# A fused attention and two-FFN kernel: the order of the loads and of the work in its first two tiles

## What is computed

```python
def _attn_ref(q, k, v, n_global, n_local):        # q, k, v: (2, 8, 768, 64)
    scores = matmul(q, k.T) / sqrt(64)
    keep = (pos_k < n_global) | ((rel >= 0) & (rel < n_local))      # 8 and 96
    scores = scores - slope[h] * dist ; scores = where(keep, scores, -1e9)
    return matmul(softmax(scores), v)             # softmax with + 1e-9 in the sum

def _moe_ref(x, w_in, w_out, g_ln):               # 512 -> 1024 -> 512
    h = x @ w_in
    solu = h * softmax(h)
    ln = (solu - mean) / sqrt(var + 1e-6) * g_ln
    return ln @ w_out

def _moe2_ref(x, w_gate, w_val, w_out, rms_g):    # 512 -> 1536 -> 512
    xn = x / rms(x) * rms_g
    return (silu(xn @ w_gate) * (xn @ w_val)) @ w_out
```

## Time and profile before

| what | value |
|---|---|
| time, median of 3 runs | 598.04 us (596.92 to 598.3) |
| span of the profiled execution, first to last instruction | 596.7 us |
| PE busy | 566.4 us, 95% of the span |
| DVE, ACT, POOL busy | 305.0, 258.1, 74.6 us |
| DMA | 46.95 MB, mean 79 GB/s |

### The profile page before, as it was taken

How to read it: one execution, slowest core, us unless ns; L and a number is a source line. 1 busy time by engine, 2 the same in 40 slices (tenths; PEclk the granted TensorE clock), 3 DMA queues, 4 the chain that set the end, 5 groups by cost and what they waited for, 6 DMA issues and landing times.

```text
span 596.7 us, 10660 instructions
## 1 busy us (share of the span) xinstructions
PE 566.4 (95%) x3696; PEld 511.4 (86%) x3696; DVE 305.0 (51%) x786; ACT 258.1 (43%) x597; POOL 74.6 (13%) x215
## 2 busy tenths in 40 slices
PE   2488999999999999999999999999999999999997
PEld 1477888888888888878899999999999999999996
DVE  5478788777877898868455223222222222231211
ACT  2566756655665677646454212221222222222112
POOL 1240220222112205213010010001001000100000
PEclk9998799999999999999999999999999999999999
DMA  7676464433443343232532100010020000000000
GB/s 171 185 192 163 132 182 125 121 101 101 124 113 103 105 126 96 83 135 82 176 109 93 49 23 2 1 70 1 1 70 0 0 0 35 0 0 36 2 1 36
DMA packets 22965, 46.95 MB, mean 79 GB/s; under 512 B 4128, under 2 KB 4128, under 8 KB 22928
## 3 DMA queue, kind: packets, MB, share of 16 engines
q1 hardware_dynamic: 22928, 46.48, 26.8%
HBM read 40.18 MB, written 6.29 MB: 78 GB/s over the span
## 4 chain that ended last, share of the span: by engine, by line
PE 78%; DVE 9%; DMA 3%; issue 3%; POOL 3%; ACT 2%; SPq 1%; ACTq 0%; DVEq 0%
PE hidden L396 9%; PE hidden L397 8%; PE hidden L398 8%; PE mixed L1211 5%; PE mixed L396 3%; PE mixed L397 3%; PE scores_b L396 3%; PE scores_b L397 3%; PE scores_b L398 3%; PE mixed L398 3%; PE turned L396 3%; PE turned L397 3%; PE scores_a L397 3%; PE turned L398 3%; PE scores_a L396 3%
## 5 line engine op out<-in xcount | busy, mean ns | idle before, releaser
L708 ACT ACTIVATE act_hi<-act_sb 128x256 fp32r<-128x256 f32 x72 | 30.1, 418 | 108.7 <-DVE act_sb L1070 108.7
L1211 PEld LDWEIGHTS mixed<-v_in,probs_t 116*128 116x128 f32 x384 | 55.3, 210 | 14.5 <-ACT probs_t L659 10.8
L1211 PE MATMUL mixed<-v_in,probs_t 116*128 116x64 f32 x384 | 54.2, 289 | 9.8 <-ACT probs_t L659 9.8
L1070 DVE TENSOR_TENSOR act_sb<-mixed,silu 128x256 f32<-128x256 f32 x36 | 15.3, 425 | 93.7 <-PE mixed L398 93.1
L1070 DVE TENSOR_TENSOR act_sb<-turned,silu 128x256 f32<-128x256 f32 x36 | 15.3, 424 | 89.0 <-PE turned L398 86.5
L396 PE MATMUL hidden<-down_hi,act_hi 128*128 128x512 f32 x144 | 57.0, 396 | 0.1
L397 PE MATMUL hidden<-down_lo,act_hi 128*128 128x512 f32 x144 | 56.9, 395 | 0.0
L398 PE MATMUL hidden<-down_hi,act_lo 128*128 128x512 f32 x144 | 56.7, 394 | 0.0
L659 ACT ACTIVATE probs_t<-turned 116x512 f32<-116x512 f32 x48 | 28.7, 597 | 60.7 <-PE turned L1196 60.7
L1075 DVE TENSOR_TENSOR act_lo<-act_sb,act_hi 128x256 fp32r<-128x256 f32 x72 | 30.6, 425 | 34.9 <-ACT act_hi L708 34.9
L649 ACT ACTIVATE probs<-logits,neg_max 128x232 f32<-128x232 f32 x96 | 45.7, 482 | 5.8 <-DVE neg_max L961 5.8
(11 more groups left out here) (140 smaller groups left out, 1537.2 us busy)
## 6 DMA issues: line engine op xcount, KB each, us to landing
qk_raw<-qk_pairs SPq DMA_DIRECT2D x96, 180.0 KB, 3.5
v_in<-v_windows SPq DMA_DIRECT2D x12, 464.0 KB
staging<-w_gate SPq DMA_DIRECT2D x3, 1024.0 KB, 6.5
staging<-w_val SPq DMA_DIRECT2D x3, 1024.0 KB, 5.5
y_spill<-y_out SPq DMA_DIRECT2D x12, 256.0 KB, 8.4
staging<-w_down SPq DMA_DIRECT2D x3, 1024.0 KB, 5.5
y_in<-y_spill SPq DMA_DIRECT2D x6, 512.0 KB, 3.7
out<-o_sb SPq DMA_DIRECT2D x12, 256.0 KB, 2.1
```

The costliest lines, as they stand in the source:

```text
L708: nc.scalar.activation(act_hi[:, slot], act_sb[:, slot], ACT.Copy).then_inc(act_rounded, 1)
L1070: nc.vector.tensor_tensor(act_sb[:, slot], val_ps[slot][:, 0:WIDE], silu[:, slot], ALU.mult).then_inc(act_ready, 1)
L1211: ins = pe.matmul(mixed[:, head * d:(head + 1) * d], probs_t[:, p % 2, h, half], v_in[:, even, half, head * d:(head + 1) * d], start=(half ...
```

## The change

The changed kernel computes the same with the same instructions, but for three things. The scales are loaded as rows (12 rows of 128 floats), PE transposes them once and ACT copies them to columns (`gain_cols`). The values come in two DMAs for each tile, of 112 and 4 partitions. And the lists are in another order at the beginning:

- SP loads all four pairs of tile 0 first, then the values, block 0, two pairs of tile 1, block 1. The bounds and the scales are issued by ACT, on its own queue, ahead of ACT's first instruction.
- Blocks 0 and 1 of `w_in` are no longer rounded and split one half after each pair of tile -1. Block 0 is done whole after its last pair, block 1 whole after the first pair of tile 0, and block 2's halves one pair later than before.
- PE no longer makes the scores of n = 4 inside tile -1. At the head of tile 0 it now transposes `x`, makes the scores of n = 4, and then all 12 products of `ffn_in(0, ..., 0, ...)`, before the pairs of tile 1 go on. ACT and DVE have the matching steps there. Products for n = 1 stay at pair 2 of tile 0.

```diff
-        round_1 = {(-1, 0): [(0, 0)], (-1, 1): [(0, 1)], (-1, 2): [(1, 0)], (-1, 3): [(1, 1)],
-                   (0, 0): [(2, 0)], (0, 1): [(2, 1)], (1, 0): [(3, 0)], (1, 1): [(3, 1)],
+        round_1 = {(-1, 3): [(0, 0), (0, 1)], (0, 0): [(1, 0), (1, 1)],
+                   (0, 1): [(2, 0)], (0, 2): [(2, 1)], (1, 0): [(3, 0)], (1, 1): [(3, 1)],
...
+        split_1[-1, 3] = split_1.pop((0, 0))
...
-                sp.dma_start(v_in[:, even], v_windows[a].rearrange("p (a n) -> p a n", a=2)
-                             ).then_inc(v_loaded[even], 16)
+                window = v_windows[a].rearrange("p (a n) -> p a n", a=2)
+                for rows in (slice(0, V_ROWS), slice(V_ROWS, HALF)):
+                    sp.dma_start(v_in[rows, even], window[rows]).then_inc(v_loaded[even], 16)
...
-            for i, n in enumerate((n_global, n_local)):
-                sp.dma_start(bounds_i[:, i, :], n.bitcast(I32).partition_broadcast(P)).then_inc(bounds_in, 16)
-            load_qk(0, 0)
-            load_qk(0, 1)
+            for p in range(pairs):
+                load_qk(0, p)
             load_v(0, 0)
             load_block(sp, 0)
-            load_qk(0, 2)
-            load_qk(0, 3)
+            load_qk(1, 0)
+            load_qk(1, 1)
             load_block(sp, 1)
-            with nc.allow_non_contiguous_dma(reason="the gains as columns"):
-                sp.dma_start(gln_col[:], g_ln.rearrange("(k p) -> p k", p=P)).then_inc(cols_loaded, 16)
-                sp.dma_start(rms_col[:], rms_g.rearrange("(k p) -> p k", p=P)).then_inc(cols_loaded, 16)
...
+            for i, n in enumerate((n_global, n_local)):
+                act.dma_start(bounds_i[:, i, :], n.bitcast(I32).partition_broadcast(P)).then_inc(bounds_in, 16)
+            act.dma_start(gain_rows[0:K1], g_ln.rearrange("(k p) -> k p", p=P)).then_inc(gains_loaded, 16)
+            act.dma_start(gain_rows[K1:], rms_g.rearrange("(k p) -> k p", p=P)).then_inc(gains_loaded, 16)
             round_qk(0, 0)
             round_qk(1, 1)
+            act.wait_ge(gains_turned, 1)
+            nc.scalar.activation(gain_cols[:], turned_x[:, 0:K1 + KM], ACT.Copy).then_inc(cols_ready, 1)
             exp_pair(0, 0, 0)
...
+                    if known(t) and t == 0 and p == 0:
+                        turn_x(t)
+                        score_pair(n, p)
+                        ffn_in(t, even, 0, range(0, KM))
                     score_pair(n + 1, (p + 1) % pairs)
...
             pe.wait_ge(ident_done, 1)
+            pe.wait_ge(gains_loaded, 32)
+            pe.transpose(turned_x[:, 0:K1 + KM], gain_rows[:], ident[0:K1 + KM, 0:K1 + KM]).then_inc(gains_turned, 1)
             score_pair(0, 0)
```

More of the change, by code:

```diff
@@ L33 @@
 HALF = WIN // 2
+V_ROWS = 112
 MASKED = 1e30
@@ L358, in round_block @@
                 return
-            act.wait_ge(cols_loaded, 32)
             for k in ks:
@@ L498, in one_tile @@
                 for p in range(pairs):
-                    if is_tile(a + 1):
+                    first = known(t) and t == 0
+                    if first and p == 0:
+                        finish_x(t, general)
+                    if is_tile(a + 1) and not (known(t) and t < 0 and p < 2):
                         load_qk(a + 1, p)
-                    if p == 1 and is_tile(t):
+                    if p == 1 and is_tile(t) and not first:
                         finish_x(t, general)
@@ L732, in one_tile @@
                     n = pairs * a + p
+                    if known(t) and t == 0 and p == 0:
+                        round_x(t, even)
+                        round_qk(n, p)
+                        round_qk(n + 1, p + 1)
+                        exp_pair(n, 1 - even, p)
                     if p == 2 and is_tile(t - 1):
                         round_ln(t - 1, 0)
-                    round_qk(n + 2, (p + 2) % pairs)
+                    if not (known(t) and t < 0 and p >= 2):
+                        round_qk(n + 2, (p + 2) % pairs)
                     if known(t) and t == tiles - 1 and p == 3:
@@ L740, in one_tile @@
                     copy_turned(n, p)
-                    if p == 0 and is_tile(t):
+                    if p == 0 and is_tile(t) and not (known(t) and t == 0):
                         round_x(t, even)
@@ L746, in one_tile @@
                         copy_y(t - DRAIN, even)
-                    exp_pair(n + 1, 1 - even if p < pairs - 1 else even, (p + 1) % pairs)
+                    if not (known(t) and t < 0 and p == 3):
+                        exp_pair(n + 1, 1 - even if p < pairs - 1 else even, (p + 1) % pairs)
                     for c, half in round_1.get((t, p), ()) if known(t) else ():
@@ L1083, in one_tile @@
                         normalise_x(t, even)
+                    if known(t) and t == 0 and p == 0:
+                        split_x(t, even)
+                        split_qk(n, p)
+                        split_qk(n + 1, p + 1)
+                        take_logits(n, 1 - even, p)
                     if p == 3 and is_tile(t):
                         max_hidden(t, 1)
-                    take_logits(n + 1, 1 - even if p < pairs - 1 else even, (p + 1) % pairs)
+                    if not (known(t) and t < 0 and p == 3):
+                        take_logits(n + 1, 1 - even if p < pairs - 1 else even, (p + 1) % pairs)
                     if p == 0 and is_tile(t - 1):
@@ L1094, in one_tile @@
                         max_hidden(t, 0)
-                    split_qk(n + 2, (p + 2) % pairs)
-                    if p == 0 and is_tile(t):
+                    if not (known(t) and t < 0 and p >= 2):
+                        split_qk(n + 2, (p + 2) % pairs)
+                    if p == 0 and is_tile(t) and not (known(t) and t == 0):
                         split_x(t, even)
@@ L1204, in mix_pair @@
                 if p == 0:
-                    pe.wait_ge(v_loaded[even], 16 * (a // 2 + 1))
+                    pe.wait_ge(v_loaded[even], 32 * (a // 2 + 1))
                 if p == 0 and (not known(a) or a >= 1):
@@ L1320, in one_tile @@
                         turn_pair(n, p)
-                        score_pair(n + 1, (p + 1) % pairs)
+                        if p < 3:
+                            score_pair(n + 1, (p + 1) % pairs)
                         mix_pair(a, 1 - even, p)
                         continue
+                    if known(t) and t == 0 and p == 0:
+                        turn_x(t)
+                        score_pair(n, p)
+                        ffn_in(t, even, 0, range(0, KM))
                     score_pair(n + 1, (p + 1) % pairs)
@@ L1328, in one_tile @@
                         turn_ln(t - 1, 0)
-                    if p in (1, 2):
+                    if p in (1, 2) and not (known(t) and t == 0 and p == 1):
                         ffn_in(t, even, p - 1, range(0, KM // 2))
@@ L1335, in one_tile @@
                     turn_pair(n, p)
-                    if p == 0:
+                    if p == 0 and not (known(t) and t == 0):
                         turn_x(t)
```

14 lines of the change are left out of this document (10 added, 4 removed).

## The result

| kernel | median, us | runs | against before (95% interval) |
|---|---|---|---|
| before, beside it | 598.3 | 5 | |
| changed | 600.85 (599.75 to 601.65) | 5 | 1.0039 (1.0021 to 1.0056) |
| before, beside the later run | 598.95 | 23 | |
| changed, once more | 601.05 (599.72 to 602.38) | 12 | 1.0040 (1.0027 to 1.0053) |

The changed kernel is 0.4% slower, by 2.1 us in the later comparison, which has more runs, and by 2.55 in the first. The time lies inside the range, 1.9 to 2.1 us above the forecast of 599.0. The difference has the sign that was forecast and is just beyond the 1.8 us that the prediction called no change. The two profiled executions lie closer together: their spans are 596.7 and 597.9, 1.2 us apart. That of the changed kernel is the fastest of its five.

A forecast was written before the change was run, and what follows sets the result against it. PE alone sets the time from tile 2's x at 81.58 us. A 9.9 us lead at tile 0's x shrinks until PE is 1.0 behind there: 598.0 + 1.0 = 599.0 us, range 595.4 to 602.2.

The forecast's parts named there:

- The DMA wait: ACT's idle 8.89 us until pair 2 of tile 0 lands at 21.13; claimed to go entirely.
- the timetable of ACT and DVE in the gap: Between tile 0's two product groups, PE waits for ACT and DVE from 39.2 to 48.1; lead left 1.3 us.
- the slower rival: At the start, bounds land 0 to 2.7 us late, one for one; middle 1.4 gives 600.4; chance with the copy 0.28.
- the rival's second half: POOL's copy at 28.2 to 30 slows block 0's split, 0.9 us at most; with late bounds 601.3; joint chance 0.28.
- The step that was mis-sized: Tile 1's x at 61.5, less 0.4, gives 61.1, 1.3 behind; small idles leave 1.0 behind at tile 2, 82.6.
- the term of 1.0: At the transpose of tile 2's x, PE is 1.0 us behind the kernel before, 82.6 against 81.58.
- the prediction's signs of being wrong: DVE's first instruction later than 5.5; n = 1 products at 0.23 from their first; tile 2's mark over 2 us off 81.58.
- bounds late or the copy in the way: Late bounds at the start or POOL's copy beside block 0's split give 600 to 602.5 us; chance 0.28.
- The clock stays up: PE's clock does not fall in tile 0's gap: 597.3 to 594, nearest 596; chance 0.17, shared with ACT and DVE faster.
- The loads are as late as before: Pair 2 of tile 0 was not late because of what stood ahead, so order helps less: 599 to 601; chance 0.03.
- its two candidates: What else could have made pair 2 of tile 0 late: the values' DMA or the scales' DMA.
- a lead of 9.9 us: Tile 0's x is transposed on PE at 30.4 instead of 40.30, a lead of 9.9 us.

The follow-up runs named there:

- the values split: The kernel before with only the values of each tile loaded in two DMAs, of 112 and 4 partitions: 591.81 us, ratio 0.9883.
- the scales as rows: The kernel before with only the scales loaded as rows on ACT's queue, transposed by PE and copied by ACT: 598.73 us, ratio 1.0002.
- all new loads: The kernel before with the change's load order, split values, and bounds and scales on ACT's queue, but the old order of work: 591.49 us, ratio 0.9881.
- the late halves: The kernel before with the changed kernel's loads and old order of work, but the halves of blocks 2 and 3 two pairs later: 597.45 us.

## Why the forecast came out as it did

**Right, step by step.** The DMA wait went entirely. Tile 0's `x` (30.4 forecast, 30.95), the first product (35.1, 35.55) and the first of n = 1 (48.1, 48.21) are within 0.6 us, so the timetable of ACT and DVE in the gap, on which the prediction rests, stood. These are the rows at its end in the changed kernel, from ACT's two halves through DVE's split to the product (timelines):

```profile
41.97 1.99 ACT L361 ACTIVATE in_hi<-staging 128x1024 fp32r<-128x1024 f32 x2
...
45.79 2.36 DVE L377 TENSOR_TENSOR in_lo<-staging,in_hi 128x1024 fp32r<-128x1024 f32 x2
```

1.9 and 2.4 were the terms, and the split ends at 48.15. The clock fell as forecast, and six of the twelve products of n = 1 cost 0.43, as forecast.

**0.5 lost early, and made up.** The bounds were 0.73 late, between the ends of 0 and 2.7, which is the first half of the slower rival. But they don't count one for one, as that rival had it: DVE waits for ACT's rounding of pair 0 too (0.34 us of idle ahead of its split at 7.32 in the kernel before, none in the changed one), and at the logits 0.30 is left. The Trainium skill's rule on queues that take turns (DMA: Bandwidth & Descriptors, Queues, rings and completion order) spoke for the lower end, and the measured 0.73 out of 0 to 2.7 agrees. A further 0.4 is POOL's copy beside block 0's split, the rival's second half, for which I allowed 0.9 at most (timelines of POOL and DVE):

```profile
25.87 1.73 POOL L567 COPY bias_even<-bias 128x1856 f32<-128x1856 f32 x1
...
27.02 2.79 DVE L377 TENSOR_TENSOR in_lo<-staging,in_hi 128x1024 fp32r<-128x1024 f32 x2 [3.60 <-ACT in_hi L361]
```

It came sooner than the 28.2 to 30 of the prediction, since the eight biases took 6.52 us and not 9.13, and lies beside the split's beginning only: 2.79 instead of 2.36. At the first product of n = 1 all but 0.1 of this was made up.

**The step that was mis-sized** is the last one. The timetable gave 61.5 for tile 1's `x`, and the row says 61.60. I then took 0.4 off, because the same timetable was 0.4 to 0.6 late for the kernel before, and a further 0.3 for small idles up to tile 2. Neither was there: PE is 1.87 behind at tile 1's `x` and 1.93 at tile 2's. That the correction came from an order in which PE had products in that stretch, and was put on one in which PE waits for DVE, is my reading of it; no run tests it. The 0.3 came back later: 1.60 behind at tile 3, 1.51 at tile 4. So the term of 1.0 was 1.9 at that mark; the spans are 1.2 apart and the medians 2.1. Two of the prediction's signs of being wrong were missed by little: DVE's first instruction is at 5.45, where the sign began at 5.5, and the mark at tile 2 is 1.93 us off, where it began at 2. The rest of the distance to 599.0 is the reference: the forecast was added to a median of 598.04 from three runs, and beside the changed kernel the kernel before took 598.3 and 598.95.

**The chances.** The rival "bounds late or the copy in the way" had the right time, 600 to 602.5, but not by its mechanism, of which 0.1 us reached the second group. "The clock stays up" is out by the windows: the clock fell, and holding it up in tile 0 gives 2.5 us, more than the 1.7 worked out for it in both tiles. "The loads are as late as before" is out by the rows; which of its two candidates had made the pair late, open in the prediction, is settled by the values split and the scales as rows.

**What the prediction said and did not draw.** It had a lead of 9.9 us at tile 0's `x` and gave it away step by step in the gap. The runs confirm both halves, with their sizes at the end: loads 7.4 us faster, order of work 9.6 slower. It never asked what the kernel would do with the loads alone, and there lay the faster kernel.

## What to carry over

A change that moves loads and work together is two changes: lay out a timetable for each alone, since here a gain of 7.4 us and a loss of 9.6 showed as 0.4%. Work that fits into an engine's waits, as the block halves did in tile -1, costs little where it stands; before it is moved, look what will then be late, on the next tile as well. And a timetable is better corrected only with an error measured in a stretch that is bound by the same engine; this last is a reading of one miss, and no run here tests it.

## What the chip showed that was not expected

- With all new loads PEclk reads 1.00 in every window from 16 to 36 us, while the matmuls have the lengths of the lower level up to 34 (scores 0.42 us at 31.3, 0.28 at 35.4). The first rise is seen in the rows only.
- The first rise is not at a fixed instant: 37.9, 37.7, 39.9 and 40.0 in four profiles alike up to there. With all new loads it was up by 35.2, and in the kernel with the late halves, alike up to there as well, the first six products cost 0.43; the first group ends 2.8 us later. Marks of single profiles can differ by as much for that reason alone.
- The values' DMA of 0.48 MB over 116 partitions, cut into 112 and 4, lets the pair behind it land 7.2 us sooner and makes the kernel 1.2% faster.
